# Routing of tokens: the plan of tiles and turns computed ahead of the rows' positions

## What is computed

```python
# x: [2304, 512], the attention's output
logits = x @ w_gate + modality_bias[modality_id]     # [2304, 8]
e_idx = np.argmax(logits, axis=1)
probs = softmax(logits)
gate_w = probs[np.arange(N), e_idx]
for e in range(8):
    mask = e_idx == e
    h = np.maximum(x[mask] @ w1[e], 0.0)             # w1[e]: 512 x 1024
    out[mask] = gate_w[mask, None] * (h @ w2[e])     # w2[e]: 1024 x 512
# dense layer behind it
h = out @ w_in                                       # 512 x 2048
y = (h * sigmoid(1.702 * h)) @ w_out                 # 2048 x 512
```

## Time and profile before

| | us |
|---|---|
| median of three runs | 1076.84 |
| lowest and highest of the three | 1074.75, 1076.89 |
| the profiled execution | 1074.59 |
| its span (first to last instruction) | 1072.9 |
| TensorE busy in it | 987.9 |
| VectorE busy in it | 484.5 |

### The profile page before, as it was taken

One profiled execution on the slowest core, in us unless ns is written; L12 is line 12 of the kernel. 1 busy time (PEld: TensorE's weight loads), 2 busy tenths in 40 slices (PEclk: granted clock), 3 DMA queues, 4 the chain that ended last, 5 costly groups with the idle time before them and its releaser, 6 DMA issues.

```text
span 1072.9 us, 19901 instructions
## 1 busy us (share of the span) xinstructions
PE 987.9 (92%) x6496; PEld 879.9 (82%) x6497; DVE 484.5 (45%) x1076; ACT 444.0 (41%) x1004; POOL 258.6 (24%) x360
## 2 busy tenths in 40 slices
PE   6999999999996269999999999999999999999994
PEld 5787787787774269999999899989999999999994
DVE  6877877877886551111111515542322323223221
ACT  4777877887874041111111415432222222222221
POOL 5665565565540121111111210001010010100101
PEclk8999999999999579999999999999999999999998
DMA  3232222222211381111111344210010000100000
GB/s 79 48 68 55 61 61 54 61 61 54 66 23 24 102 269 46 38 36 39 39 39 39 111 130 142 68 50 30 2 59 0 29 29 0 59 0 0 30 1 30
DMA packets 103422, 57.18 MB, mean 53 GB/s; under 512 B 84917, under 2 KB 93659, under 8 KB 103387
## 3 DMA queue, kind: packets, MB, share of 16 engines
q1 hardware_dynamic: 92072, 40.15, 13.9%
q0 software_dynamic: 4224, 10.51, 3.2%
q10 hardware_dynamic: 7091, 6.08, 1.7%
HBM read 41.49 MB, written 15.22 MB: 53 GB/s over the span
## 4 chain that ended last, share of the span: by engine, by line
PE 81%; DVE 6%; issue 5%; POOL 4%; ACT 1%; DMA 1%; DVEq 1%; ACTq 0%; POOLq 0%; SPq 0%
PE s_ps L1395 18%; PE s_ps L1378 12%; PE s_ps L1332 11%; PE o_ps L1239 7%; PE pt_ps L1378 6%; PE o_ps L1345 6%; PE s_ps L1225 5%; PE misc L1345 5%; PE pt_ps L1191 5%; DVE probs L715 2%; PE pt_ps L1205 2%; PE pt_ps L1323 2%; DVE tile_x L895 1%; POOL qk_parts L578 1%; POOL k_swap L588 1%
## 5 line engine op out<-in xcount | busy, mean ns | idle before, releaser
L978 DVE TENSOR_TENSOR g<-s_ps,sig 128x384 f32<-128x384 f32 x96 | 53.5, 558 | 279.3 <-ACT sig L1162 279.3
L1162 ACT ACTIVATE sig<-s_ps 128x384 f32<-128x384 f32 x96 | 47.2, 492 | 273.5 <-PE s_ps L1395 273.5
L760 DVE TENSOR_SCALAR_CACHE_REDUCE scores<-s_ps,taus 128x576 f32<-128x576 f32 x144 | 117.8, 818 | 61.7 <-PE s_ps L1225 39.2
L715 DVE SCALAR_TENSOR_TENSOR probs<-scores,thresh,probs 128x576 f32<-128x576 f32 x144 | 131.1, 911 | 0.0
L1191 PE MATMUL pt_ps<-ident,probs 128*128 128x128 f32 x720 | 126.9, 278 | 3.5 <-ACT pT L1001 1.9
L1395 PE MATMUL s_ps<-yT_high,w_in_high 128*128 (+1 forms) x384 | 129.5, 337 | 0.3 <-issue 0.2
L1395 PE MATMUL s_ps<-yT_high,w_in_low 128*128 (+1 forms) x384 | 129.5, 337 | 0.0
L1395 PE MATMUL s_ps<-yT_low,w_in_high 128*128 (+1 forms) x384 | 129.0, 336 | 0.0
L669 POOL DMA_INDIRECT out_dram<-out_sb,table x18 | 18.9, 1050 | 422.6 <-ACT out_sb L1137 418.9
L1038 ACT ACTIVATE probs<-scores,row_low 128x576 f32<-128x576 f32 x144 | 115.5, 802 | 10.2 <-DVE scores L760 8.5
L908 DVE SCALAR_TENSOR_TENSOR hT_low<-s_ps,hT_high 128x512 fp32r<-128x512 f32 x40 | 27.6, 692 | 177.7 <-ACT hT_high L1082 177.7
(11 more groups left out here) (209 smaller groups left out, 2228.2 us busy)
## 6 DMA issues: line engine op xcount, KB each, us to landing
w_raw<-in_moe_w_dram SPq DMA_DIRECT2D x16, 512.0 KB, 4.6
yT_dram<-tile_yT ACTq DMA_DIRECT2D x11, 512.0 KB, 2.9
x_dram<-xs SPq DMA_DIRECT2D x32, 128.0 KB, 2.0
w_in_raw<-in_moe_w_in_dram SPq DMA_DIRECT2D x4, 1024.0 KB, 5.3
w_out_raw<-in_moe_w_out_dram SPq DMA_DIRECT2D x16, 256.0 KB, 2.6
qk<-in_k_dram SPq DMA_DIRECT2D x30, 128.0 KB, 2.4
next_yT<-yT_dram SPq DMA_DIRECT2D x5, 768.0 KB, 4.5
qk<-in_q_dram SPq DMA_DIRECT2D x16, 128.0 KB, 2.1
```

Of the source, the lines that this page charges most:

```text
L715: dve.scalar_tensor_tensor(out=probs[:, i % PROB_SLOTS, 0:SEQ], in0=scores[:, i % SCORE_SLOTS], scalar=thresh[:, j, u:u + 1], in1=probs[:, ...
L760: dve.tensor_scalar(scores[:, i % SCORE_SLOTS].rearrange("p (c n) -> p c n", c=2), s_ps[i % 2][:, :, 0:HALF], taus[:, 3:4], None, ALU.mult ...
```

## The change

The plan block (L848 to L884 before, L822 to L858 after) is moved ahead of the place block, on VectorE alone. No instruction is added, removed or altered; the two copies of the table stay behind both. The programs of the other four engines are as before.

```diff
             link(dve.tensor_tensor(rows_first[:], rows_end[:], rows_of_expert, ALU.subtract))
-            dve.wait_ge(split_ready, 1)
-            link(dve.tensor_tensor(place_e[:], rank_ps[:, 0:RT * E].rearrange("p (t e) -> p t e", e=E),
-                                   earlier[:].rearrange("p e t -> p t e"), ALU.add))
...
-            dve.tensor_tensor(slot_tok[:], slot_hot[:], by_token(token_id[:], RT), ALU.mult
-                              ).then_inc(one_hot_ready, 1)
-            dve.tensor_tensor(row_hot[:], by_token(place_row[:], P), iota_row[:].unsqueeze(1).to_broadcast([P, RT, P]),
-                              ALU.is_equal).then_inc(one_hot_ready, 1)
-
-
             def per_expert(ap, n):
                 return ap.unsqueeze(1).to_broadcast([1, n, E])
...
             link(dve.tensor_reduce(plan[:, PL_NEAR:PL_NEAR + 1], near[:], AX.X, ALU.add))
             dve.tensor_copy(plan_i[:], plan[:]).then_inc(plan_ready, 1)
+
+            dve.wait_ge(split_ready, 1)
+            link(dve.tensor_tensor(place_e[:], rank_ps[:, 0:RT * E].rearrange("p (t e) -> p t e", e=E),
+                                   earlier[:].rearrange("p e t -> p t e"), ALU.add))
...
+            dve.tensor_tensor(slot_tok[:], slot_hot[:], by_token(token_id[:], RT), ALU.mult
+                              ).then_inc(one_hot_ready, 1)
+            dve.tensor_tensor(row_hot[:], by_token(place_row[:], P), iota_row[:].unsqueeze(1).to_broadcast([P, RT, P]),
+                              ALU.is_equal).then_inc(one_hot_ready, 1)
+
             dve.wait_ge(table_written, 1)
             dve.tensor_copy(order_sq[:, 0:RT], table_ps).then_inc(order_ready, 1)
             dve.tensor_copy(table[:], table_ps).then_inc(table_ready, 1)
```

## The result

| | before | after |
|---|---|---|
| median of five runs, us | 1075.13 | 1081.1 |
| lowest and highest | 1074.46, 1076.89 | 1080.38, 1083.92 |
| the profiled execution, us | 1074.59 | 1081.1 |
| its span, us | 1072.9 | 1079.5 |

The changed kernel takes 1.0057 times as long as the kernel before (95% interval 1.0038 to 1.0075): 6 us slower, where 4.9 were forecast. On the page the busy times of all engines agree within 0.2 us but for 1.7 us more on POOL, so the loss is waiting.

A forecast was written before the change was run, and what follows sets the result against it. Matmul time bounds most of the kernel; between attention and experts VectorE's chain through table and first gather does. +4.1 for exposed table matmuls and +0.8 for weight traffic give +4.9, 1076.84 to 1081.7 us, range 1078.0 to 1084.0.

The forecast's parts named there:

- The lost cover: Table matmuls between attention and experts: no longer hidden under the plan block, so `order_sq` starts 4.1 us later.
- The earlier weights: SP's weight loads: first weight issued at 359.0 instead of 364.74, 5.7 us earlier, bringing nothing in the sum.
- the wait holds up nobody else: VectorE's queue behind its table wait: copies, cast and scaling all serve the same chain, so no other engine is delayed.
- Contention: First tile's gather: meets more weight traffic, so its last landing comes 0.8 us later, kept between -0.9 and +1.5.
- the upper bound that I used: First gather's landing: likened to the second tile's gather inside the weight stream, gates 4.8 and 5.0 us, making +1.5.
- the cap of +0.5: First gather: with VectorE idle, 1.02 us of extra issue time would not recur, so the traffic term tops at +0.5.
- The clock: TensorE in some tiles: one more or fewer dip of the granted clock shifts any case by 1.5 us; no chance given.
- rival D: First gather: w2 pieces and both row gathers land together, full price or more, +5.6 to +7 us; chance 0.12.
- main case: Path to the first `up`: later table plus slower gather, +4.9 us, 1081.7 us; chance 0.70.
- A: First `up`: waits for w1 weights, not the gather, so an earlier plan gains up to 5.7 us, 1071.1; chance 0.04.
- B: Between table and `up`: some wait swallows the exposed 4.1 us, time stays 1076.8; chance 0.06.
- Rival C: First gather: runs without weight traffic, landing in 2.6 us, so +3.2 us in all, 1080.0; chance 0.08.

The follow-up runs named there:

- two kernels without weight traffic: Changed kernel and kernel before, each with SP waiting for the first tile's gather before loading any weights: ratios 1.0064 and 1.0020 of the kernel before.
- the doubling: The 18 table matmuls made twice, in the kernel before and in the changed kernel: 1.0041 and 1.0096 of the kernel before.
- changed kernel with early increments: Changed kernel with VectorE's two starting increments for SP moved from behind the table's copies to directly behind `plan_i`: 1.0056 of the kernel before.
- changed, increments early, w2 held: Changed kernel with both starting increments directly behind `plan_i` and SP waiting for the first gather between w1 and w2: 1.0027 of the kernel before.
- table in pieces, mid plan: Kernel before with `row_hot` in three pieces, each releasing six table matmuls, and the table copied mid plan behind L866: 0.9956, 1070.94 us.
- before, increments early: Kernel before with the two starting increments for SP moved directly behind `plan_i`, nothing else: 1.0017 of the kernel before.
- table mid plan: Kernel before with the table's wait and two copies moved into the plan block behind L874, the stored order's cast a little later: 1.0008.

## Why the prediction came out as it did

**The lost cover** was right, as worked out: +4.1 forecast, +4.16 measured at `order_sq` and again between the two kernels without weight traffic; the doubling shows the mechanism.

**The earlier weights** failed in the step "SP issues its first weight at 359.0". I had taken `plan_ready` for the only thing that SP waits for. Its load has a second wait, for the low parts of the expert before (`w1_low_ready`), which for the first expert is fed by the increment at L928, behind the table's copies in VectorE's queue. The order of VectorE's instructions shown with the change ends just ahead of it, and so did my list of what is queued behind the new wait: "all serve that same chain, so the wait holds up nobody else" was false: it held up SP for 8.8 us. For ACT this cost nothing, since the weights had slack. But it put the start of the weights 0.26 us ahead of the gather, and the changed kernel with early increments shows the price: there the last gate lands after 3.87 us instead of 5.36, and `up` starts 1.36 us earlier. In that run, the case that the prediction had assumed, `up` is 4.66 us behind the kernel before (44.11 against 39.45). The 1.36 us cover what the forecast lacked at `up` (6.0 against 4.9).

**Contention** had the right sign and the wrong size: +0.8, measured +1.86 in the first pair and 2.1 in the second. The working assumed a stream that had run for 9 us. In fact weights and gather started 0.26 us apart. Where the assumed case was made, the landing took 3.87 us, which is +0.4 on the kernel before. So the upper bound that I used, the second tile's gather at 5.0, was close to what happened (5.36 and 5.57, above it), for a reason other than mine. In the changed kernel POOL's last issue took 0.94 us with VectorE idle, and the gate landed after 5.4 us all the same, so slow issue is not what made it late. The Trainium skill, "SBUF — State Buffer", section "SBUF: two separate sides", says that a DMA issued by GpSimd can be late because VectorE, in a two-port operation, keeps it from writing descriptors; the cap of +0.5 that I drew from it is refuted by that row, though not the page's sentence itself, which no run here tests. The slow issues do come back: in the changed kernel's second gather the last three, from 385.26 on, took 1.96 to 1.97 us, inside VectorE's `w_low` run (384.04 to 393.21), which the prediction had seen in one row only. One of the issues that it took for partly inside that run, at 378.82 before, lay wholly inside and took 1.10. ACT was splitting weights for most of the same time, so which engine slows them is not shown.

**The clock** stood among the rivals as 1.5 us a dip, with no side taken. That was right: one more drop and a slower first `up` are nearly all of the 2.5 us between the two profiles of the kernel before, and between the two compared above, with five drops each, the clock adds only 0.4 us (see below).

**The sum**: 4.9 forecast, 6.0 between medians, 6.5 between the profiled executions. Between the profiled executions 1.6 us are missing: 1.1 in the contention term, 0.4 behind the start of `up`, and 0.1 in the routing's later start. At `up` the shift of +6.0 lies where rival D had put it (+5.6 to +7), not in the main case's middle. That agreement is luck, for D's reason was w2 pieces beside the row gathers, and the first w2 piece went out only at 377.51, when the last gate landed (377.6). Rivals A and B are out: earlier weights alone brought nothing but a quicker gather, and nothing between table and `up` took up the 4.2 us. Rival C's price, a gather alone, is what the held-back runs measured, 2.55 us, but it is not what the change makes. In absolute terms the 1081.7 came closer (1081.1) than the parts deserve: I added to 1076.84, the median of three runs, and the median of five is 1075.13.

## What to carry to other kernels

When two independent blocks on one queue are exchanged, ask which of them releases work on another engine that this queue later waits for: that block goes first and the other one covers the wait. List everything that stands behind a wait on its engine, bare semaphore increments included; they are easy to miss and can hold a third engine. And an earlier transfer is only worth what it does for its consumer, while the moment at which its pieces go out beside a short gather on the critical path made 1 to 3 us here.

## What the runs showed of the hardware that was not expected

**How long a gather takes beside a weight stream goes with the moment at which a piece of weights is issued.** First weight minus first gather issue; the issues of weight pieces nearest to that of the last gate, before (-) and behind (+) it; and the last gate's landing from its issue to the scaling:

| kernel | weights start behind gather, us | nearest pieces, us from the last gate's issue | landing, us |
|---|---|---|---|
| weights held back (two kernels) | after landing | +3.53, +3.54 | 2.55, 2.56 |
| changed, increments early, w2 held | -9.17 | -8.30, +2.66 | 2.62 |
| table in pieces, mid plan | 5.04 | +0.95, +1.52 | 2.92 |
| before, twice | 0.81, 0.80 | -2.6, +1.4 | 3.50, 3.46 |
| changed, increments early | -9.16 | -2.11, +1.43 | 3.87 |
| before, doubled | -0.26 | -0.93, +2.83 | 4.85 |
| before, increments early | 0.69 | -2.74, +0.32 | 4.89 |
| changed, doubled | -0.25 | -0.96, +2.99 | 5.02 |
| table mid plan | 3.45 | -0.52, +0.04 | 5.08 |
| changed, twice | -0.26, -0.26 | -0.84 and +0.78, -0.91 and +0.74 | 5.36, 5.57 |

The start of the weights alone does not order the landings: 0.81 and 0.69 us stand 1.4 us apart. The third column does. Wherever the landing took 4.8 us or more, a piece of weights had been issued between 0.96 us before and 0.32 us behind the last gate; in the others none was between 2.1 us before and 0.9 us behind it. In the kernel before SP issued the third piece 1.44 us behind the last gate. With early increments the first piece landed after 3.45 us instead of 4.46, so the third went out 0.32 us behind the gate. SP's timeline from the third piece on, in the kernel before (last gate's issue at 367.91) and then with early increments (last gate's issue at 367.73):

```profile
369.35 1.64 SPq L521 DMA_DIRECT2D w_raw<-in_moe_w_dram  x2
```
```profile
368.05 2.19 SPq L521 DMA_DIRECT2D w_raw<-in_moe_w_dram  x2
```

This was read from the profiles afterwards; no run moved one piece alone, and only the kernel before and the changed one were profiled twice. What happens in the DMA engines is open.

**TensorE's clock drops for short stretches between tiles, in every kernel here.** In the expert stage TensorE waits 2.2 us at each tile for the next one's scaling, and behind some of these waits the granted clock is 0.50 (1.2 GHz) for 3 to 4 us; one such drop costs 1.5 us. In the kernel before (columns as in the earlier trace rows):

```profile
449.00:451.00 2.00, 0.00 (x0) 0.00 (x0) 1.34 (x3) 0.60 (x1) 0.00 (x0) 1.00 0.00 0
451.00:453.00 2.00, 1.80 (x10) 1.80 (x11) 0.49 (x2) 0.70 (x2) 0.00 (x0) 0.64 0.00 0
453.00:455.00 2.00, 2.00 (x12) 2.00 (x10) 1.04 (x2) 0.48 (x1) 1.00 (x2) 0.50 0.00 0
455.00:459.00 4.00, 4.00 (x35) 4.00 (x35) 0.00 (x0) 0.00 (x0) 2.81 (x3) 1.00 0.43 130
```

Five of the ten tiles' turns are hit so in its first profile, six in its second, and the stretch from `up` to the end of the span is 690.00 and 692.50 us: the same kernel, 2.5 us apart. Of this, 1.5 us are the sixth drop and 0.8 are in the first `up`, which begins at the lower clock (13.46 and 14.27 us here). All eleven other profiles of the study lie between 690.1 and 692.8, and the granted clock sorts them: with five drops behind the first `up` the stretch takes 690.0 to 690.4 us, with six or seven 691.9 to 692.8. That is as large as most of the effects in this study, so that effects of 1 to 2 us had to be read from positions ahead of `up`, and the run with early increments, 1.4 us ahead at `up`, showed no gain in time.
